# One core, attention and two MLP stages: low parts of the squares on VectorE alone, two weight splits moved

## The reference

```python
def _moe2_ref(x, mu_k, mu_r, w_k, w_v, w_r):
    x_prev = np.concatenate([np.zeros((B, 1, D)), x[:, :-1, :]], axis=1)
    xk = mu_k * x + (1.0 - mu_k) * x_prev
    xr = mu_r * x + (1.0 - mu_r) * x_prev
    k = np.maximum(xk @ w_k, 0.0)           # w_k: 320 x 1024
    v = k * k @ w_v                         # w_v: 1024 x 320
    r = 1.0 / (1.0 + np.exp(-(xr @ w_r)))   # w_r: 320 x 320
    return (r * v)
```

## Time and profile before

| | |
|---|---|
| median of 3 runs | 343.88 us (343.7 to 344.51) |
| the profiled execution | 343.79 us |
| its span, first to last instruction | 342.1 us (1.69 us lie around it) |
| PE busy | 323.0 us, 94% of the span |
| DVE busy | 212.1 us, 62% |
| ACT busy | 141.6 us, 41% |
| POOL busy | 68.8 us, 20% |
| mean granted PE clock | 0.980 |

### The profile page before, as it was taken

One profiled execution on the slowest core, in us unless ns is written; L12 is line 12 of the kernel. 1 busy time (PEld: TensorE's weight loads), 2 busy tenths in 40 slices (PEclk: granted clock), 3 DMA queues, 4 the chain that ended last, 5 costly groups with the idle time before them and its releaser, 6 DMA issues.

```text
span 342.1 us, 5769 instructions
## 1 busy us (share of the span) xinstructions
PE 323.0 (94%) x2112; PEld 307.8 (90%) x2112; DVE 212.1 (62%) x448; ACT 141.6 (41%) x272; POOL 68.8 (20%) x94
## 2 busy tenths in 40 slices
PE   8879969999999999977999999999799999999996
PEld 4769869999899989857999999999699999999996
DVE  7775798557565566645274278988669635855111
ACT  5954474333323332272211254438775246426100
POOL 8612222112112200060112030113123003003000
PEclk9888999999999999999899999999899999999999
DMA  6970331123314213500000501012000100010011
GB/s 207 278 224 9 81 80 40 41 80 81 79 39 135 80 40 130 180 2 0 1 2 5 179 2 56 5 50 104 2 0 0 40 20 3 19 40 0 19 40 57
DMA packets 9816, 20.94 MB, mean 61 GB/s; under 512 B 1789, under 2 KB 5389, under 8 KB 9309
## 3 DMA queue, kind: packets, MB, share of 16 engines
q1 hardware_dynamic: 9788, 20.58, 20.2%
HBM read 18.53 MB, written 1.97 MB: 60 GB/s over the span
## 4 chain that ended last, share of the span: by engine, by line
PE 76%; DVE 14%; issue 4%; ACT 4%; POOL 1%; DVEq 0%; ACTq 0%; POOLq 0%
PE ps_v L1060 17%; PE ps_s L1060 10%; PE ps_e L1060 7%; PE ps_in L1060 6%; PE ps_out L1060 6%; PE ps_t L1060 6%; PE ps_in L1139 5%; PE ps_out L1149 5%; PE ps_s L1130 5%; PE ps_z L1060 4%; PE ps_z L1158 2%; PE ps_e L1106 1%; DVE kr L1032 1%; PE ps_e L1111 1%; DVE pt L791 1%
## 5 line engine op out<-in xcount | busy, mean ns | idle before, releaser
L526 POOL TENSOR_TENSOR kkl<-kr,kkh 128x384 fp32r<-128x384 f32 x16 | 17.6, 1098 | 73.4 <-ACT kkh L681 73.4
L1032 DVE TENSOR_TENSOR kr<-kr 128x384 f32<-128x384 f32 x32 | 20.4, 641 | 14.5 <-ACT kr L724 14.4
L1130 PEld LDWEIGHTS ps_s<-qkt 128*128 128x128 f32 x192 | 26.3, 203 | 1.5
L1130 PE MATMUL ps_s<-qkt 128*128 128x128 f32 x192 | 27.2, 287 | 0.0
L561 ACT ACTIVATE et<-ps_e 128x512 f32<-128x512 f32 x24 | 14.3, 596 | 29.0 <-PE ps_e L1111 20.9
L1139 PEld LDWEIGHTS ps_in<-tok,pt 128*128 128x128 f32 x192 | 24.1, 191 | 1.4
L1139 PE MATMUL ps_in<-tok,pt 128*128 128x42 f32 x192 | 24.7, 279 | 0.0
L697 ACT ACTIVATE gh<-ut 128x384 fp32r<-128x384 f32 x16 | 8.4, 525 | 34.9 <-DVE ut L997 34.9
L1060 PE MATMUL ps_v<-win,xth 128*128 128x512 f32 x60 | 20.8, 411 | 1.3 <-DVE xtl L866 1.3
L521 POOL TENSOR_TENSOR gl<-ut,gh 128x384 fp32r<-128x384 f32 x8 | 9.5, 1188 | 60.1 <-ACT gh L697 60.1
L1060 PE MATMUL ps_v<-xth,win 128*128 128x384 f32 x65 | 19.1, 359 | 2.5 <-ACT vr L567 1.4
(11 more groups left out here) (293 smaller groups left out, 926.6 us busy)
## 6 DMA issues: line engine op xcount, KB each, us to landing
tok<-in_vk SPq DMA_DIRECT2D x12, 328.0 KB, 4.8
qkt<-in_qk SPq DMA_DIRECT2D x12, 320.0 KB
sp_raw<-in_w_sp SPq DMA_DIRECT2D x6, 384.0 KB, 5.1
osig<-in_og SPq DMA_DIRECT2D x2, 960.0 KB, 10.5
out_y<-ob SPq DMA_DIRECT2D x12, 160.0 KB, 1.8
wv_raw<-in_w_v SPq DMA_DIRECT2D x2, 640.0 KB, 4.9
win_raw<-in_w_in SPq DMA_DIRECT2D x4, 256.0 KB, 8.0
wk_raw<-in_w_k SPq DMA_DIRECT2D x2, 512.0 KB, 4.0
```

The lines of the kernel that those rows point to most:

```text
L526: gp.tensor_tensor(kkl[a % 2][:, b, :], kr[n % 4][:, :], bits(kkh[a % 2][:, b, :]), ALU.subtract).then_inc(sems["kk_lo_pool"], 1)
L1032: ve.tensor_tensor(kr[n % 4][:, :], kr[n % 4][:, :], kr[n % 4][:, :], ALU.mult).then_inc(sems["kk_done"], 1)
L1130: last = te.matmul(ps_s[j][:, h * CH:(h + 1) * CH], qkt[:, u % NS, 1, cols], qkt[:, u % NS, 0, cols], start=True, stop=True)
```

## The change

It makes three edits. The low parts of all squares go to DVE, each right after the next square (POOL makes none). w_r is split during sp(3,1) and sp(3,2), and its two full-height low parts are made by POOL. The high parts of w_v are made by ACT at k(0,3) to k(0,6), its low parts by DVE at r(0,2) and y(2,TA), y(2,TB), y(2,TL).

```diff
+WV_LO = {("r", 0, 2): (0,), ("y", 2, TA): (1,), ("y", 2, TB): (2,), ("y", 2, TL): (3,)}
...
 (POOL)
-                if kind == "k" and b % 2 == 0:
-                    n = 8 * a + b
-                    pool.wait_ge(sems["kk_hi_done"], n + 1)
-                    gp.tensor_tensor(kkl[a % 2][:, b, :], kr[n % 4][:, :], bits(kkh[a % 2][:, b, :]),
-                                     ALU.subtract).then_inc(sems["kk_lo_pool"], 1)
+                if key == ("sp", 3, 2):
+                    for t in range(2):
+                        pool.wait_ge(sems["wr_hi"], 2 + t)
+                        gp.tensor_tensor(wr[:, 2 + t, :], wr_raw[:, t, :], bits(wr[:, t, :]),
+                                         ALU.subtract).then_inc(sems["wr_lo"], 1)
...
 (ACT)
+                    if (a, b) == (3, 1):
+                        left_hi(wr, wr_raw, "wr_in", 64, "wr_left", "wr_hi")
+                    if (a, b) == (3, 2):
+                        rows_hi(wr, wr_raw, "wr_left_lo", "wr_hi")
...
-                    if n == 0:
-                        left_hi(wr, wr_raw, "wr_in", 64, "wr_left", "wr_hi")
-                        rows_hi(wr, wr_raw, "wr_left_lo", "wr_hi")
...
-                        act.wait_ge(sems["kk_lo_pool"], (n - 4) // 2 + 1)
-                        act.wait_ge(sems["kk_lo_dve"], (n - 4 + 1) // 2)
+                        act.wait_ge(sems["kk_lo_dve"], n - 3)
...
-                    if a == 1 and 1 <= b <= 4:
-                        f = 2 * (b - 1)
+                    if a == 0 and 3 <= b <= 6:
+                        f = 2 * (b - 3)
                         act.wait_ge(sems["wv_in"], 32)
+                        act.wait_ge(sems["g_lo_pool"], 2 * NBLK)
+                        act.wait_ge(sems["g_lo_dve"], 2 * NBLK)
                         sc.activation(wv_hi[:, f:f + 2, :], ...)
...
 (DVE)
+                    if (a, b) == (3, 1):
+                        left_lo(wr, wr_raw, "wr_left", "wr_left_lo")
...
-                    if n == 0:
-                        left_lo(wr, wr_raw, "wr_left", "wr_left_lo")
-                        rows_lo(wr, wr_raw, "wr_hi", "wr_lo")
...
-                    if b in (2, 4, 6):
+                    if b > 0:
                         square_lo(n - 1)
...
-                    if a == 1 and 2 <= b <= 5:
-                        f = 2 * (b - 2)
-                        ...
+                for i in WV_LO.get(key, ()):
+                    f = 2 * i
+                    dve.wait_ge(sems["wv_hi_done"], i + 1)
+                    ve.tensor_tensor(wv_lo[f // 4][:, f % 4:f % 4 + 2, :], wv_raw[f // 4][:, f % 4:f % 4 + 2, :],
+                                     bits(wv_hi[:, f:f + 2, :]), ALU.subtract).then_inc(sems["wv_lo_done"], 1)
```

More of the change, by code:

```diff
@@ L144 @@
 gate_m gate_next gates_in group_mm gwt_done head_rows_done ident_done ident_zero later_done later_zero ones_done k_relu
-kk_done kk_hi_done kk_lo_dve kk_lo_pool kw_done mix_biased mix_gated mrow_in
+kk_done kk_hi_done kk_lo_dve kw_done mix_biased mix_gated mrow_in
 mu_done mu_in nm_hi_done nm_zero nm_lo_done num_done o_in0 o_in1 osig_done out_done0 out_done1 out_ready
@@ L1037, in _ @@
                         square_lo(n)
-                    if a == 1 and 2 <= b <= 5:
-                        f = 2 * (b - 2)
-                        dve.wait_ge(sems["wv_hi_done"], b - 1)
-                        ve.tensor_tensor(wv_lo[f // 4][:, f % 4:f % 4 + 2, :], wv_raw[f // 4][:, f % 4:f % 4 + 2, :],
-                                         bits(wv_hi[:, f:f + 2, :]), ALU.subtract).then_inc(sems["wv_lo_done"], 1)
+                for i in WV_LO.get(key, ()):
[3 more added lines that the diff above has]
+                                     bits(wv_hi[:, f:f + 2, :]), ALU.subtract).then_inc(sems["wv_lo_done"], 1)
                 if kind == "v":
@@ L1303, in _ @@
                         pe.wait_ge(sems["kk_hi_done"], 8 * a + 8)
-                        pe.wait_ge(sems["kk_lo_pool"], 4 * a + 4)
-                        pe.wait_ge(sems["kk_lo_dve"], 4 * a + 4)
+                        pe.wait_ge(sems["kk_lo_dve"], 8 * a + 8)
                     t_ = slice(b * CH, b * CH + CH)
```

## The result

The changed kernel takes 348.55 us (median of 15 runs), the kernel before 344.41 us in the same comparison (15 runs). The ratio is 1.0084, 95% interval 1.0049 to 1.0119: slower by 0.84%, about 2.9 us (1.7 to 4.1). The ratio leaves out the executions in the chip's slower state, three of the changed kernel and one of the kernel before; the medians of the others are 346.99 and 344.1 us. The time from there to the end of the span is called the list.

A forecast was written before the change was run, and what follows sets the result against it. The prediction took PE's one wait, 2.35 us before k(1,0), plus its clock loss of 1.67, to bound the kernel. Its terms -1.76 + 0.33 + 2.55 gave +1.12, so 343.79 became 344.9 us, range 343.0 to 346.0.

The forecast's parts named there:

- sum of +1.12: Shift of PE's start of k(1,0): -1.76 + 0.33 + 2.55, giving 344.9 us; forecast chance 0.45.
- What bounds the kernel: PE's single wait in the list, 2.35 us before k(1,0), is the only place to gain, unless the change makes another.
- the 4.0 that I had put on the gap: Cost of the wait before k(1,0): 2.35 us of waiting plus 1.67 of lowered clock behind it.
- w_r's left tile, +1.47: At sp(3,1) DVE's left subtraction waits for ACT's copy, starting shift 7 1.47 us later, not absorbed within sp(3).
- POOL's two tiles: POOL's two full w_r subtractions at sp(3,2) hold up DVE; the sp(3,3) gate ends 2.55 us late in all.
- rival of POOL holding on: DVE not let in between POOL's instructions, gate 3.3 us late, or w_v data late: 345.6 us; chance 0.17.
- POOL being harmless: POOL's two subtractions do not hold up DVE; gate 1.47 us late, sum +0.04, 343.8 us; chance 0.18.
- w_r leaves k(0,0), D passed on: Without four w_r copies relu(0) starts 1.76 us earlier, but the sp(3,3) gate's delay (D, 2.55) is passed on whole.
- The loop of k(0), +0.33: From relu(0) to shift 10, 10.13 us instead of 9.80, ACT setting the pace at 1.41 a round with w_v copies.
- The w_v data: Load issued behind the last gate lands at 235.7, in time by 0.4 us for ACT's first w_v copy in k(0).
- The clock loss of 1.67 I leave as it is: Low clock behind the wait before k(1,0) costs 1.67 us as before, with bounds of -0.3 and +0.2.
- The faster rival: DVE not late in sp(3), gate delay 0: 342.4 us, or 340.7 if the clock stays up; chance 0.15.

The follow-up runs named there:

- e4: Kernel before with all squares' low parts on DVE and shifts 10 and 11 moved forward to k(0,3) and k(0,5): ratio 0.9896.
- e12: e4 run again unchanged on another chip: ratio 0.9910 against the kernel before, list 115.05 us.
- e6: Changed kernel with POOL's two w_r subtractions given back to DVE at k(0,0): one run, list 119.50 us.
- e5: Changed kernel with DVE's left w_r subtraction, ACT's full copies and POOL's subtractions one group later each: one run, list 119.22 us.
- e11: Changed kernel run again unchanged on another chip: ratio 1.0107 against the kernel before, list 120.12 us.
- e1: Kernel before with only the squares' low parts all moved to DVE: ratio 0.9947, list 116.07 us.
- e3: Changed kernel with w_v split in k(1) again, keeping the squares' and w_r's moves: ratio 0.9955 against the kernel before.
- e9: Kernel before with only shifts 10 and 11 moved forward to k(0,3) and k(0,5): ratio 0.9955, list 116.90 us.
- e2: Changed kernel with w_r split at k(0,0) again on ACT and DVE: ratio 1.0025 against the kernel before.
- e7: Kernel before with w_r's move alone: one run, list 119.34 us.
- e10: Kernel before with w_v's move alone: one run, list 121.18 us.

## Why the prediction was right and wrong

The sign, the place and the mechanism of the wait were right, the size was too small: 344.9 forecast, +0.3%, against +0.84% (1.0049 to 1.0119). My sum of +1.12 lies under the interval of 1.7 to 4.1, and the measured medians above my range of 343.0 to 346.0. In the profile of the change the +2.54 are 0.39 more of wait and 1.03 more of clock than the sum had; the step that failed is the one on the clock.

- *What bounds the kernel*: right. The one wait is the only place where the time changed, and e4 and e12 take it away and have 4.0 us less of list, the 4.0 that I had put on the gap.
- *w_r's left tile, +1.47*: measured +1.67 (ACT starts the left copy 0.55 after the gate's, not 0.43). *POOL's two tiles*: the gate ends 2.45 late, forecast 2.55. DVE is let in between, so the rival of POOL holding on falls, and so does the one of POOL being harmless (e6 against the change: 0.75 at the gate). What I put down in favour of the latter, that `scaled` is not touched by POOL, is wrong as well: beside POOL it took 1.03 in e5, and 1.06 at 204.92 already in the trace of the kernel before. The Trainium skill's figure ("GPSIMD Engine Reference", section 3.1: about 2.6 cycles an element, as an estimate 0.69 for 320 elements) is too low here: e5's pair took 0.92 for each.
- *w_r leaves k(0,0), D passed on*: relu(0) forecast 0.79 late, was 0.57 late.
- *The loop of k(0), +0.33*: the rounds of 1.41 are there. **The w_v data** were not in time by 0.4 but late by 0.46 in the profile, which made the loop +0.94. In e11 the first copy starts 3.37 after relu(0) and not 3.71, and the wait is 3.55, against the 3.5 forecast. This step was too near its edge to be costed at nothing: the landing time is 4.8 in e11 and 5.2 in the other profile of the same kernel, and of the 0.34 between the two copies' starts 0.31 went into PE's wait. So the late data, which I had only as a rival, came true in one profile.
- ***"The clock loss of 1.67 I leave as it is"***: this is the step that failed. I set its bounds at -0.3 and +0.2. In the profile it was 2.70, +1.03. The fall did come at the same time as before, one of my two cases, and 1.07 of the low stretch lay in the gap; but the clock was low for 6.8 and not for 3.4. In w_v alone (wait 3.41) k(1) lost 2.79 by its length, while waits of 2.35 to 3.10 lost 1.40 to 1.60 and that of 3.55 (e11) lost 1.57. A wait of this length can thus cost one low stretch of 3.4 or one of twice that, and a sum has to carry the second as a case. In e11, where it is 3.4, the list is 1.12 longer than before, which is my sum; in the other profile of the change it is 2.53 longer. That the sum came out to the hundredth in e11 is partly luck: its wait is 1.20 longer and its clock costs 0.03 less.
- *The faster rival* ("the work goes where DVE has time", 342.4 or 340.7) has fallen for the change as made, but its mechanism was seen: where the wait is 1.05 or 1.57 (e1, e3), the clock stays up and 1.6 comes back at once.

What stays open: the ratio's 2.9 us lie above both profiles of the change, which differ from before by 1.12 and 2.53 in the list; the interval's lower end, 1.7, lies between them. How often the long low stretch comes, two profiles can't say, and of the kernel before there is one profile only. I have no other place in the list that changed, and the attention part starts and ends alike but for its clock; whether that clock is touched by the change I cannot tell from two profiles.

## What to carry to other kernels

Where one wait of PE is the end of a chain that runs through two queues, move first the instructions PE waits for, not the load in front of them: two entries of a table took 2.1 us off the list (119.00 to 116.90), where the two moved splits added to it, and with the squares on DVE it is 115.03. Work moved forward out of a busy place must find its operands ready and its engine idle where it goes; on an engine that is already late it is paid again, and everything that hangs behind it, a DMA's issue too, is late with it. And a wait on PE has to be priced with the clock behind it, which came in steps here, nothing, 3.4 us or 6.8 us at half clock: from 2.35 to 1.57 it gave back 0.8 of waiting and 1.6 of clock.

## What the runs showed of the hardware

The same wait does not always have the same clock behind it. Ahead of sp(0,0) PE waits 2.0 us in every kernel here; in twelve of the fourteen profiles the clock then fell to 0.50 for some 3.4 us and sp(0) to k(0,0) took 63.06, in two (e9, e11) it stayed at 1.00 and took 61.51, with the same instructions. These are two stretches of e9, to hold against the same place in the kernel before, whose stretches follow:

```profile
161.00:162.00 1.00, 1.00 (x6) 1.00 (x7) 0.00 (x0) 0.00 (x0) 0.00 (x0) 1.00 0.00 0
162.00:163.00 1.00, 1.00 (x8) 1.00 (x7) 0.00 (x0) 0.00 (x0) 0.00 (x0) 1.00 0.00 0
```

```profile
161.00:162.00 1.00, 1.00 (x4) 1.00 (x4) 0.00 (x0) 0.00 (x0) 0.00 (x0) 0.50 0.00 0
162.00:163.00 1.00, 1.00 (x5) 1.00 (x5) 0.00 (x0) 0.00 (x0) 0.00 (x0) 0.50 0.00 0
```

Behind the wait before k(1,0) the low stretches have two lengths: 3.4 in the kernel before, e2, e5, e6, e7 and e11, and 6.8 in the change and e10. In the two long ones the clock had fallen 1.07 and 0.73 before PE resumed; in the six others it fell at most 0.41 before PE resumed, or up to 1.50 after. These are eight profiles, and what makes the difference they do not show.

And between 10 and 30 us the clock is low for longer in one execution than in another (its mean there is 0.83 in the kernel before, 0.58 in the change; in e1 and e10 it is also low for some time between 40 and 60 us), so that sp(0,0) starts anywhere from 160.0 to 162.9. The same kernel can do either: the change starts it at 162.41 in one profile and at 160.97 in the other. So single runs can lie 3 us apart by this alone, whatever the kernel.
